# LSH attention and two expert layers on one core: q and k transposed side by side, hashed by three products a half, and placed by copies inside SBUF

## The chip, the cores and the metric

The kernel runs on one core of a Trainium2 chip. The metric is the device time of one execution in microseconds (us), the median of several runs; lower is better. Beside the runs one execution was profiled.

## The reference

The kernel computes an attention with a hashing mask and two mixture-of-experts layers behind it. The attention is what matters here. It has 2 x 8 = 16 heads, 768 positions and a head width of 64, all in float32:

```python
B, H, S, D = q.shape                     # 2, 8, 768, 64
q_bits = (np.einsum('bhsd,dk->bhsk', q, proj) > 0)     # proj: 64 x 6
k_bits = (np.einsum('bhsd,dk->bhsk', k, proj) > 0)
mask = q_bucket[:, :, :, None] == k_bucket[:, :, None, :]   # all 6 bits equal
scores = scale * np.matmul(q, k.transpose(0, 1, 3, 2))
scores = np.where(mask, scores, -1000000000.0)
attn = softmax(scores)                   # over the keys
out = np.matmul(attn, v)
```

Its result, 1536 tokens of 512 values, goes through two expert layers (8 experts each, the first with the two best experts of a token, the second with the best one).

## The kernel before

**Split values.** TensorE multiplies here in a float32 form of reduced precision (F32R). Where float32 exactness is wanted, a value is split into a high part (its rounded copy) and a low part (what is left), and the products high x high, high x low and low x high are summed.

**Operands of the scores.** Scores need q and k with the head width on the partitions. A head has four operand tiles of 128 x 768, in two sets (parity of the head): `q_hl` (rows 0 to 63 high part of q, rows 64 to 127 low part), `k_hh` (high part of k twice), `q_hb` and `k_lb` (rows 0 to 63 high part of q and low part of k; rows 64 to 75 the hash bits as large or tiny numbers, so that positions of different buckets get a huge negative score). One half of a score tile is two products: `q_hl` x `k_hh`, and `q_hb` x `k_lb` over 76 rows.

**Preparing a head.** `load_qk` on the SP queue brings k and q in twice each (four DMAs in 256-byte pieces), so that each is side by side with itself. Six units, listed in `PREP`, turn them: ("k", 0), ("q", 0), ("k", 1), ("q", 1), then ("bits", 0), ("bits", 1); the number is the half of the 768 positions. A k or q unit is three transposes of 128 x 128 on TensorE into a PSUM bank (`prep_unit`, L1024), a copy of the high part by ACT (`copy_unit`, L548) and the subtraction that gives the low part on DVE (`prep_unit`, L696). As k or q stands there twice, the bank has it in rows 0 to 63 and again in rows 64 to 127, so each engine writes every piece straight to the rows where it belongs; only the high part of q in `q_hl` is a copy by GpSimd (`q_copy`, L448). A bits unit is four hashing products into the bank (108 rows: the bits of k in rows 64 to 75, those of q in 96 to 107) and two comparisons on DVE.

**The head's steps.** A head has 6 tiles of 128 queries, one for each step j. In step j TensorE issues (L1096): the scores of tile j, the unit j of the next head, the weighing (`weigh`, probabilities x v) of the tile two back, and the transposes of the probabilities (`turn`) of the tile before. DVE (L752) finds the tile's maximum and the two scalars of its exponential (L722 to L728), does its part of the unit and every second time half of an evacuation; ACT (L579) does its part of the unit, the exponential of tile j, then the evacuations of the turned probabilities. The scores' banks and the operand sets are double.

**The SP queue** issues in its own order (L362 to L370), for each head: wait for the four transpose units, load q and k of the head after next; wait for the last weighing of the head before, load v. After every second head come `clear` twice and `clear_y`: zeros to tables in HBM, 2.6 MB in three DMAs. Semaphores: `qk_ld` loads landed, `prep_mm` a unit on TensorE done, `prep_cp` a high part copied, `prep_ev` a unit on DVE done, `q_top` GpSimd's copy done.

Of the kernel before, what the change touches and what calls it, by code (L numbers as in the profile page):

```python
# [5 lines left out]
P = 128  # L6
# [14 lines left out]
def lsh_attention_two_moes(nc, q, k, v, proj, moe_w_gate, moe_w_noise, moe_noise, moe_w1, moe_w2,  # L21
# [31 lines left out]
    with ctx:  # L53
# [16 lines left out]
        qraw = raw[:, 0:2].rearrange("p a t d -> p (a t d)").rearrange("p (t r d) -> p t r d", t=QT, d=D)  # L70
        kraw = raw[:, 2:4].rearrange("p a t d -> p (a t d)").rearrange("p (t r d) -> p t r d", t=QT, d=D)
# [12 lines left out]
        k_lb = [ring_part(3), ring_part(7)]  # L84
        probs = [work[:, i * S:(i + 1) * S] for i in range(2)]
# [27 lines left out]
        p_f = work[:, 0:2 * PW].rearrange("p (a b) -> p a b", a=2)  # L113
        p_h, p_l = (ring_part(8 + i)[:, 0:2 * PW].rearrange("p (a b) -> p a b", a=2) for i in range(2))
        p_k1 = ring_part(10)[:, 0:PW]
# [92 lines left out]
        prep_cp = sem("prep_cp")  # L208
        prep_ev = sem("prep_ev")
        q_top = sem("q_top")  # L210
# [81 lines left out]
        PREP = [("k", 0), ("q", 0), ("k", 1), ("q", 1), ("bits", 0), ("bits", 1)]  # L292
        U = len(PREP)
        assert QT == U

# [28 lines left out]
        def _(sp):  # L324
            def load_qk(h):
                for raw_rows, t in ((kraw, k), (qraw, q)):
                    for r in range(2):
                        sp.dma_start(raw_rows[:, :, r], head_rows(t, h)).then_inc(qk_ld, 16)

            def load_v(h, par):  # L330
                sp.dma_start(vraw[:, par], head_rows(v, h)).then_inc(v_ld[par], 16)

# [22 lines left out]
            sp.wait_ge(prep_mm, 4)  # L355
            load_qk(1)
            sp.wait_ge(pool_c, 1)
# [75 lines left out]
        def _(pool):  # L433
# [13 lines left out]

            def q_copy(h, par):  # L448
                for half in range(2):

                    pool.wait_ge(prep_cp, h * 4 + (2 * half + 2))
                    high = q_hb[par][0:D, cols(half)].bitcast(F32)
                    nc.gpsimd.tensor_tensor(q_hl[par][0:D, cols(half)], high, ones[0:D, 0:1].broadcast_to([D, HALF]),  # L453
                                            ALU.mult).then_inc(q_top, 1)

            q_copy(0, 0)
            over_heads(pool, lambda h, par: None if last(h) else q_copy(h + 1, 1 - par))
# [78 lines left out]
        def _(act):  # L536
# [7 lines left out]
            act.wait_ge(qk_ld, 64)  # L544
# [3 lines left out]
            def copy_unit(h, par, u):  # L548

                what, half = PREP[u]  # L550
                if what in ("k", "q"):
                    act.wait_ge(prep_mm, h * U + (u + 1))
                    to = k_hh[par] if what == "k" else q_hb[par]
                    nc.scalar.activation(to[:, cols(half)], prep_bank(h, u)[:, 0:HALF],  # L554
                                         ACT.Copy).then_inc(prep_cp, 1)
# [19 lines left out]

            for u in range(U):
                copy_unit(0, 0, u)

            def head(h, hp):  # L579
                for j in range(QT):  # L580
                    n = h * QT + j
                    if not last(h):
                        copy_unit(h + 1, 1 - hp, j)
# [75 lines left out]
        def _(dve):  # L659
# [23 lines left out]
            link(vec.tensor_scalar(bit_rule[:, 3:4], second[:], -2.0, 1.0, ALU.mult, ALU.add))  # L683
            link(vec.memset(p_f, 0.0))
            dve.wait_ge(proj_ld, 32)

            for side in range(2):
                neg, plus = (QB, QB + BITS) if side == 0 else (D + BITS, D)
                link(vec.tensor_scalar(p_f[:, side, neg:neg + BITS], praw[:], -1.0, None, ALU.mult))
                link(vec.tensor_copy(p_f[:, side, plus:plus + BITS], praw[:]))  # L690
            link(vec.tensor_copy(p_h, p_f))
            link(vec.tensor_tensor(p_l, p_f, p_h.bitcast(F32), ALU.subtract))
            link(vec.tensor_copy(p_k1[0:D, :], p_h[0:D, 1, :]))
            link(vec.tensor_copy(p_k1[D:P, :], p_l[D:P, 1, :]))

            def prep_unit(h, par, u):  # L696
                what, half = PREP[u]
                c = cols(half)
                bank = prep_bank(h, u)
                if what == "k":  # L700
                    dve.wait_ge(prep_cp, h * 4 + (u + 1))
                    ins = vec.tensor_tensor(k_lb[par][0:D, c], bank[0:D, 0:HALF],
                                            k_hh[par][0:D, c].bitcast(F32), ALU.subtract)
                elif what == "q":
                    dve.wait_ge(prep_cp, h * 4 + (u + 1))
                    ins = vec.tensor_tensor(q_hl[par][D:P, c], bank[D:P, 0:HALF],
# [603 lines left out]
```

## Time and profile before

| | |
|---|---|
| median of 3 runs | 1034.82 us (1034.65 to 1037.06) |
| profiled execution | 1035.75 us, its span 1033.9 us, mean granted clock 0.96 |
| TensorE matmuls busy | 936.5 us, 91% of the span |
| DVE, ACT, GpSimd busy | 587.9, 340.3, 410.1 us |
| attention | first scores at 16.95 us, last at 340.3 us |
| DMA | 158.3 MB, 153 GB/s over the span |

The profile is one execution. An instruction's row has its start from the span's start, its duration, engine, line and operands; PE is TensorE's matmul, PEld its weight load, DVE VectorE, ACT ScalarE, POOL GpSimd, SPq the queue of SyncE that issues DMAs. Brackets tell how long an engine sat idle before and what ended that. Matmul durations overlap, so starts are what to compare. The granted clock is TensorE's, 1.00 being 2.4 GHz and 0.50 being 1.2 GHz.

### The profile page before, as it was taken

What the parts mean: (1) busy time and instruction counts of PE and PEld (TensorE: products, weight loads), DVE (VectorE), ACT (ScalarE), POOL (GpSimd) and SP (SyncE); (2) the same over time, 40 slices, a digit from 0 to 9 for tenths busy, and PEclk for the clock granted to TensorE, in tenths of its full rate; (3) what the DMA queues carried; (4) which work ended last, traced back from release to release, by engine and by line L of the source; (5) the groups of instructions that cost most, each with busy time, mean ns of one, the idle gap of its engine ahead of it and who ended that gap; (6) DMA issues with size and microseconds to landing.
All of it is one profiled execution on the core that took longest, in us unless ns stands there. A gap on an engine that the chain in (4) does not pass through costs nothing. (4 is left out here: it accounts for less than half of the span.)

```text
span 1033.9 us, 19204 instructions
## 1 busy us (share of the span) xinstructions
PE 936.5 (91%) x5502; PEld 793.0 (77%) x5503; DVE 587.9 (57%) x1136; ACT 340.3 (33%) x548; POOL 410.1 (40%) x251
## 2 busy tenths in 40 slices
PE   6999999999999938999999999999854999999980
PEld 4889988988898726888888888888643788888860
DVE  5777777777777474544445544454367454444432
ACT  2655555565555410422121111120212134342000
POOL 1000000000000547966152433331955889896004
PEclk9999999999999967999999999999976999999995
DMA  8351543435514525655252534332765677774107
GB/s 264 95 156 38 147 138 70 139 89 124 142 38 171 203 98 207 238 191 189 75 181 84 170 102 141 122 131 87 231 210 189 216 239 254 234 252 147 47 31 243
DMA packets 116173, 158.31 MB, mean 153 GB/s; under 512 B 57904, under 2 KB 59952, under 8 KB 116144
## 3 DMA queue, kind: packets, MB, share of 16 engines
q1 hardware_dynamic: 83280, 70.37, 22.3%
q10 hardware_dynamic: 26624, 67.12, 19.9%
q0 software_dynamic: 6240, 20.45, 6.1%
q8 instruction: 16, 0.26, 0.1%
q14 instruction: 13, 0.11, 0.0%
HBM read 104.43 MB, written 53.48 MB: 153 GB/s over the span
## 5 line engine op out<-in xcount | busy, mean ns | idle before, releaser
L463 POOL TENSOR_TENSOR wring<-stage,wring 128x1024 f32 (+1 forms) x128 | 302.3, 2395 | 197.1 <-ACT wring L618 197.0
L618 ACT ACTIVATE wring<-stage 128x1024 f32 (+1 forms) x128 | 135.4, 1061 | 429.7 <-POOL wring L463 213.8
L1203 PE MATMUL bank<-wring,xT_hl 128*128 x352 | 142.7, 405 | 5.2 <-DVE xT_hl L936 5.2
L1083 PE MATMUL bank<-raw,work 128*128 128x64 f32 x1152 | 143.6, 275 | 3.2 <-ACT work L569 3.2
L1083 PEld LDWEIGHTS bank<-raw,work 128*128 128x128 f32 x1152 | 135.9, 191 | 12.9 <-issue 10.9
L1220 PE MATMUL bank<-wring,hT_hl 128*128 x352 | 141.6, 402 | 3.2 <-DVE hT_hl L955 3.2
L453 POOL TENSOR_TENSOR wring<-wring,ones 64x384 fp32r<-64x384 f32 x32 | 26.2, 819 | 287.3 <-ACT wring L554 287.3
L1205 PE MATMUL bank<-wring,xT_hl 128*128 x352 | 138.8, 394 | 0.0
L1204 PE MATMUL bank<-wring,xT_hl 128*128 x352 | 137.9, 392 | 0.0
L1222 PE MATMUL bank<-wring,hT_hl 128*128 x352 | 137.8, 391 | 0.0
L1221 PE MATMUL bank<-wring,hT_hl 128*128 x352 | 137.1, 390 | 0.0
L962 DVE COPY work<-bank 128x512 f32<-128x512 f32 x44 | 30.5, 694 | 178.2 <-PE bank L1222 168.5
L561 ACT ACTIVATE work<-bank,stat 128x768 f32<-128x768 f32 x96 | 95.2, 991 | 101.8 <-DVE stat L728 101.8
L722 DVE TENSOR_REDUCE stat<-bank 128x1 f32<-128x768 f32 x96 | 91.8, 956 | 59.7 <-PE bank L1060 58.5
L943 DVE TENSOR_SCALAR work<-bank 128x512 f32<-128x512 f32 x88 | 60.9, 692 | 108.2 <-PE bank L1205 108.2
L1203 PEld LDWEIGHTS bank<-wring,xT_hl 128*128 128x128 f32 x352 | 66.8, 190 | 18.6 <-issue 6.2
L1071 PE MATMUL bank<-ident,work 128*128 128x128 f32 x576 | 79.9, 275 | 0.6 <-ACT work L569 0.6
L1220 PEld LDWEIGHTS bank<-wring,hT_hl 128*128 128x128 f32 x352 | 66.1, 188 | 16.1 <-issue 3.7
L1205 PEld LDWEIGHTS bank<-wring,xT_hl 128*128 128x128 f32 x352 | 66.6, 189 | 14.8
L1222 PEld LDWEIGHTS bank<-wring,hT_hl 128*128 128x128 f32 x352 | 66.1, 188 | 14.7
L1204 PEld LDWEIGHTS bank<-wring,xT_hl 128*128 128x128 f32 x352 | 67.0, 190 | 13.0
L1221 PEld LDWEIGHTS bank<-wring,hT_hl 128*128 128x128 f32 x352 | 66.3, 188 | 12.7
(171 smaller groups left out, 1290.6 us busy)
## 6 DMA issues: line engine op xcount, KB each, us to landing
stage<-in_moe_w_dram ACTq DMA_DIRECT2D x128, 512.0 KB, 4.0
ys<-work SPq DMA_DIRECT2D x44, 256.0 KB, 3.4
work<-xs SPq DMA_DIRECT2D x40, 256.0 KB, 3.5
xs<-stage SPq DMA_DIRECT2D x7, 1024.0 KB, 4.5
ys<-stage SPq DMA_DIRECT2D x7, 1024.0 KB, 8.2
raw<-in_k_dram SPq DMA_DIRECT2D x32, 192.0 KB, 3.6
raw<-in_q_dram SPq DMA_DIRECT2D x32, 192.0 KB, 3.8
xs<-stage SPq DMA_DIRECT2D x7, 512.0 KB, 5.2
```

The lines of the kernel that those rows point to most:

```text
L463: nc.gpsimd.tensor_tensor(wring[:, bass.ds(at + DC * F, GW)], stage[:, j % STAGES, :], wring[:, bass.ds(at, GW)].bitcast(F32), ALU.subtrac ...
L561: nc.scalar.activation(probs[par].rearrange("p (b c) -> p b c", b=2), s_ps[par][:, :, 0:HALF], ACT.Exp, bias=stat[:, par, 2:3], scale=stat ...
L618: nc.scalar.activation(wring[:, bass.ds(parity * SLOT + high_at(j), GW)], stage[:, j % STAGES, :], ACT.Copy).then_inc(w_high, 1)
L722: vec.tensor_reduce(stat[:, par, 0:1], s_ps[par][:, :, 0:HALF], AX.XY, ALU.max).then_inc(s_max, 1)
L1071: ins = nc.tensor.transpose(pt_ps[:, half, i * P:(i + 1) * P], probs[par][:, c:c + P], ident[:])
L1083: ins = mm(o_ps[:, j * D:(j + 1) * D], probsT[j % 2][:, i * P:(i + 1) * P], vraw[:, hp, i], start=i == 0, stop=i == QT - 1)
L1203: mm(o, xT_hl[:, 0, c, :], wh, start=c == 0, stop=False)
L1204: mm(o, xT_hl[:, 0, c, :], wl, start=False, stop=False)
L1205: ins = mm(o, xT_hl[:, 1, c, :], wh, start=False, stop=c == DC - 1)
L1220: mm(y_ps[:], hT_hl[:, 0, c, :], wh, start=c == 0, stop=False)
L1221: mm(y_ps[:], hT_hl[:, 0, c, :], wl, start=False, stop=False)
L1222: ins = mm(y_ps[:], hT_hl[:, 1, c, :], wh, start=False, stop=c == FC - 1)
```

## The change

- q and k are loaded once each, side by side in `qk_raw` (q in columns 0 to 63, k in 64 to 127): two DMAs a head instead of four.
- One unit for each half transposes both: q comes to rows 0 to 63, k to rows 64 to 127. ACT copies the high parts to `qk_top`, DVE subtracts to `qk_rest`, each 128 x 768 and single, not double.
- A bits unit has three products of 128 rows, `p_h` x `qk_top`, `p_h` x `qk_rest`, `p_l` x `qk_top`, and one comparison of 44 rows into `k_lb`, which carries the bits of q along in rows 96 to 107.
- A head has four units (`U = 4`), in steps 0 to 3; steps 4 and 5 have none.
- Seven DMAs inside SBUF (`put`) on the SP queue place the pieces: six of 64 rows x 768 when both subtractions are done, one of 12 rows (the bits of q) when both comparisons are. `qk_put` counts them; the first scores of a head wait for all seven and for the head's four units.
- The SP queue's order for a head is: wait, six copies, q and k of the head after next, wait, seventh copy, wait, v. The clears stay behind every second head.
- GpSimd's `q_copy` is gone. The bits rule and the projections are laid out for the new rows (DVE, at the start).

```diff
-        qraw = raw[:, 0:2]...
-        kraw = raw[:, 2:4]...
+        qk_raw = raw[:, 0:2].rearrange("p a t d -> p (a t d)").rearrange("p (t x) -> p t x", x=2 * D)
+        qk_top = ring_part(11)
+        qk_rest = ring_part(12)
...
-        PREP = [("k", 0), ("q", 0), ("k", 1), ("q", 1), ("bits", 0), ("bits", 1)]
-        U = len(PREP)
+        U = 4
+        PUTS = 7
...
             def load_qk(h):
-                for raw_rows, t in ((kraw, k), (qraw, q)):
-                    for r in range(2):
-                        sp.dma_start(raw_rows[:, :, r], head_rows(t, h)).then_inc(qk_ld, 16)
+                for at, t in ((0, q), (D, k)):
+                    sp.dma_start(qk_raw[:, :, at:at + D], head_rows(t, h)).then_inc(qk_ld, 16)
...
+            def put(to, at, n, t, row):
+                sp.dma_start(to[at:at + n, :].bitcast(F32), t[row:row + n, :].bitcast(F32)).then_inc(qk_put, 16)
+
+            def put_split(h, par):
+                sp.wait_ge(prep_ev, h * U + 2)
+                put(q_hl[par], 0, D, qk_top, 0)
+                put(k_hh[par], 0, D, qk_top, D)
+                put(q_hl[par], D, D, qk_rest, 0)
+                put(k_hh[par], D, D, qk_top, D)
+                put(q_hb[par], 0, D, qk_top, 0)
+                put(k_lb[par], 0, D, qk_rest, D)
+
+            def put_bits(h, par):
+                sp.wait_ge(prep_ev, h * U + 4)
+                put(q_hb[par], D, 2 * BITS, k_lb[par], QB)
...
-            sp.wait_ge(prep_mm, 4)
+            put_split(0, 0)
             load_qk(1)
+            put_bits(0, 0)
...
+            def next_head(h, par):
+                put_split(h + 1, 1 - par)
+                load_qk(h + 2)
+                put_bits(h + 1, 1 - par)
+                sp.wait_ge(s_pv, h * QT + QT)
+                load_v(h + 2, par)
+
             with sp.Fori(0, (H - 2) // 2) as i:
                 for par in range(2):
-                    sp.wait_ge(prep_mm, i * (2 * U) + (U * par + U + 4))
-                    load_qk(i * 2 + (2 + par))
-                    sp.wait_ge(s_pv, i * (2 * QT) + QT * (par + 1))
-                    load_v(i * 2 + (2 + par), par)
+                    next_head(i * 2 + par, par)
                 for m in range(2):
                     clear(m, i * share[m], share[m])
                 clear_y(0, i * share[0], share[0])
+            put_split(H - 1, 1)
+            put_bits(H - 1, 1)
...
-            def copy_unit(h, par, u):
...
+            def top_part(h, u):
+
+                act.wait_ge(prep_mm, h * U + (u + 1))
+                nc.scalar.activation(qk_top[:, cols(u)], prep_bank(h, u)[:, 0:HALF], ACT.Copy).then_inc(prep_top, 1)
...
+                if u < 2:
+                    dve.wait_ge(prep_top, h * 2 + (u + 1))
+                    ins = vec.tensor_tensor(qk_rest[:, c], bank[:, 0:HALF], qk_top[:, c].bitcast(F32), ALU.subtract)
                 else:
                     dve.wait_ge(prep_mm, h * U + (u + 1))
+                    b = slice(D, PW)
+                    ins = vec.tensor_scalar(k_lb[par][b, c], bank[b, 0:HALF], bit_rule[b, 2:3], bit_rule[b, 3:4],
+                                            ALU.is_gt, ALU.mult)
...
                     for i in range(KH):
+                        ins = nc.tensor.transpose(bank[:, i * P:(i + 1) * P], qk_raw[:, half * KH + i], ident[:])
                 else:
-                    mm(to, p_k1, k_hh[par][:, c], start=True, stop=False)
-                    mm(to, p_h[0:D, 1, :], k_lb[par][0:D, c], start=False, stop=False)
-                    pe.wait_ge(q_top, h * 2 + 2)
-                    mm(to, p_h[:, 0, :], q_hl[par][:, c], start=False, stop=False)
-                    ins = mm(to, p_l[0:D, 0, :], q_hb[par][0:D, c], start=False, stop=True)
+                    to = bank[0:PW, 0:HALF]
+                    mm(to, p_h, qk_top[:, c], start=True, stop=False)
+                    mm(to, p_h, qk_rest[:, c], start=False, stop=False)
+                    ins = mm(to, p_l, qk_top[:, c], start=False, stop=True)
...
             def scores(n, j, h, hp):
+                if j == 0:
+                    pe.wait_ge(qk_put, h * (16 * PUTS) + 16 * PUTS)
+                    pe.wait_ge(prep_ev, h * U + U)
...
-                    if not last(h):
+                    if not last(h) and j < U:
                         prep_unit(h + 1, 1 - hp, j)
```

## Rows read from the trace of the kernel before

**Rows 1.** Busy us by stage: engine (instructions), granted clock, DMA share, GB/s; attention.
```profile
200.00:250.00 50.00, 49.66 (x379) 45.56 (x379) 38.15 (x80) 29.80 (x62) 4.10 (x5) 1.00 0.34 93
```

**Rows 2.** Groups of instructions, 20 to 420 us: busy us, mean ns, idle before.
```profile
L453 POOL TENSOR_TENSOR wring<-wring,ones 64x384 fp32r<-64x384 f32 x30 | 24.6, 819 | 278.9 <-ACT wring L554 278.9
...
L710 DVE TENSOR_SCALAR wring<-bank,bit_rule 12x384 fp32r<-12x384 f32 x30 | 20.2, 674 | 1.0
```

**Rows 3.** One line's instructions: duration ns, least, median, most.
```profile
L728 DVE SCALAR_TENSOR_TENSOR stat<-stat x96: 159/160/556, 20.7 to 341.7; 128x1 f32<-128x1 f32 x96
```

**Rows 4.** Timeline, one head: start, us, engine, line; each step's first score weights.
```profile
61.04 0.19 PEld L1059 LDWEIGHTS bank<-wring 128*128 128x128 f32 x1
...
64.03 0.19 PEld L1059 LDWEIGHTS bank<-wring 128*128 128x128 f32 x1
...
70.43 0.19 PEld L1059 LDWEIGHTS bank<-wring 128*128 128x128 f32 x1
...
74.50 0.19 PEld L1059 LDWEIGHTS bank<-wring 128*128 128x128 f32 x1
...
78.58 0.19 PEld L1059 LDWEIGHTS bank<-wring 128*128 128x128 f32 x1
...
81.59 0.19 PEld L1059 LDWEIGHTS bank<-wring 128*128 128x128 f32 x1
```

**Rows 5.** Timeline: the last hashing product's weight load, and the weighing behind it.
```profile
72.20 0.17 PEld L1048 LDWEIGHTS bank<-wring 64*108 64x108 f32 x1 [0.18 <-issue]
...
72.56 1.41 PEld L1083 LDWEIGHTS bank<-raw,work 128*128 128x128 f32 x12 [0.19 <-issue]
```

**Rows 6.** Timeline: exponentials, and the weighings' weight loads.
```profile
63.91 0.99 ACT L561 ACTIVATE work<-bank,stat 128x768 f32<-128x768 f32 x1 [1.03 <-DVE stat L728]
...
65.49 1.42 PEld L1083 LDWEIGHTS bank<-raw,work 128*128 128x128 f32 x12 [0.38 <-issue]
...
79.64 1.42 PEld L1083 LDWEIGHTS bank<-raw,work 128*128 128x128 f32 x12
...
81.08 0.99 ACT L561 ACTIVATE work<-bank,stat 128x768 f32<-128x768 f32 x1 [0.64 <-DVE stat L728]
```

**Rows 7.** Timeline of the SP queue: start, us of issue, what is issued.
```profile
63.67 0.37 SPq L331 DMA_DIRECT2D raw<-in_v_dram  x1
...
64.25 1.00 SPq L352 DMA_DIRECT2D xs<-stage  x2
...
65.43 0.97 SPq L348 DMA_DIRECT2D ys<-stage  x1
...
89.48 1.25 SPq L328 DMA_DIRECT2D raw<-in_k_dram  x2
```

**Rows 8.** Single microseconds, columns as in rows 1: clears, then loads; loads alone.
```profile
66.00:67.00 1.00, 1.00 (x12) 1.00 (x11) 0.93 (x4) 0.19 (x1) 0.00 (x0) 1.00 1.03 397
...
72.00:73.00 1.00, 1.00 (x6) 0.63 (x7) 0.90 (x4) 0.11 (x1) 0.00 (x0) 1.00 0.99 221
...
76.00:77.00 1.00, 1.00 (x6) 0.63 (x6) 0.90 (x4) 0.03 (x1) 0.00 (x0) 1.00 0.39 62
...
93.00:94.00 1.00, 1.00 (x9) 0.89 (x8) 0.93 (x3) 0.55 (x1) 0.00 (x0) 1.00 1.14 257
```

**Rows 9.** DMA issues by kind: count, KB each, median us to landing.
```profile
raw<-in_v_dram SPq DMA_DIRECT2D x16, 192.0 KB, 2.4
```

**Rows 10.** Timeline: the first score product's weight load.
```profile
16.95 0.29 PEld L1059 LDWEIGHTS bank<-wring 128*128 128x128 f32 x1 [0.33 <-issue]
```

**Rows 11.** Two-microsecond slices ahead of the experts, columns as in rows 1.
```profile
368.00:370.00 2.00, 0.86 (x7) 0.44 (x4) 0.28 (x1) 0.88 (x2) 0.00 (x0) 1.00 0.00 0
...
370.00:372.00 2.00, 0.00 (x0) 0.00 (x0) 0.84 (x4) 1.99 (x4) 0.00 (x0) 0.88 0.72 260
...
396.00:398.00 2.00, 1.31 (x3) 1.12 (x4) 0.37 (x1) 0.00 (x0) 1.58 (x2) 0.50 0.51 156
...
402.00:404.00 2.00, 2.00 (x10) 1.68 (x9) 0.69 (x1) 0.00 (x0) 1.39 (x3) 0.94 0.43 164
```

More of the change, by code:

```diff
@@ L112, in lsh_attention_two_moes @@
         PW = QB + 2 * BITS
-        p_f = work[:, 0:2 * PW].rearrange("p (a b) -> p a b", a=2)
-        p_h, p_l = (ring_part(8 + i)[:, 0:2 * PW].rearrange("p (a b) -> p a b", a=2) for i in range(2))
-        p_k1 = ring_part(10)[:, 0:PW]
+        p_f = work[:, 0:PW]
+        p_h, p_l = (ring_part(8 + i)[:, 0:PW] for i in range(2))
         wg_sb = [sb("wg0", [P, DC, 2 * E]), sb("wg1", [P, DC, E])]
@@ L446, in _ @@
             nc.gpsimd.iota(tri_in[:], [[1, E], [-1, E]], base=0, channel_multiplier=0, **io).then_inc(pool_c, 1)
[L448 to L457, printed above, removed]
             def low_part(g, parity, pieces=range(GRAN)):
@@ L543, in _ @@
             AHEAD = STAGES - 2
-            act.wait_ge(qk_ld, 64)
+            act.wait_ge(qk_ld, 32)
             for j in range(AHEAD):
                 load_piece(0, 0, j)
-            def copy_unit(h, par, u):
[L550 to L555, printed above, removed]
+            def top_part(h, u):
+                act.wait_ge(prep_mm, h * U + (u + 1))
+                nc.scalar.activation(qk_top[:, cols(u)], prep_bank(h, u)[:, 0:HALF], ACT.Copy).then_inc(prep_top, 1)
             def expo(n, par, j, hp):
@@ L574, in evacs @@
                     evac(n, j % 2, 1, pt_b)
-            for u in range(U):
-                copy_unit(0, 0, u)
+            for u in range(2):
+                top_part(0, u)
             def head(h, hp):
@@ L581, in head @@
                     n = h * QT + j
-                    if not last(h):
-                        copy_unit(h + 1, 1 - hp, j)
+                    if not last(h) and j < 2:
+                        top_part(h + 1, j)
                     expo(n, j % 2, j, hp)
@@ L683, in _ @@
             link(vec.tensor_scalar(bit_rule[:, 3:4], second[:], -2.0, 1.0, ALU.mult, ALU.add))
+            link(vec.tensor_copy(bit_rule[QB:P, 2:4], bit_rule[QB:P, 0:2]))
             link(vec.memset(p_f, 0.0))
             dve.wait_ge(proj_ld, 32)
[L687 to L690, printed above, removed]
+            for rows, neg, plus in ((slice(0, D), QB, QB + BITS), (slice(D, P), D + BITS, D)):
+                link(vec.tensor_scalar(p_f[rows, neg:neg + BITS], praw[rows, :], -1.0, None, ALU.mult))
+                link(vec.tensor_copy(p_f[rows, plus:plus + BITS], praw[rows, :]))
@@ L1024, in prep_unit @@
             def prep_unit(h, par, u):
-                what, half = PREP[u]
+                half = u % 2
                 if not first(h):
@@ L1053, in scores @@
                     pe.wait_ge(s_exp, n - 1)
+                if j == 0:
+                    pe.wait_ge(qk_put, h * (16 * PUTS) + 16 * PUTS)
+                    pe.wait_ge(prep_ev, h * U + U)
                 t = slice(j * P, (j + 1) * P)
                 for half in range(2):
-                    if j == 0:
-                        pe.wait_ge(prep_ev, h * U + (U - 1 + half))
                     o, c = s_ps[j % 2][:, half, 0:HALF], cols(half)
@@ L1089, in _ @@
             pe.wait_ge(pool_c, 9)
-            for u in range(4):
+            for u in range(2):
                 prep_unit(0, 0, u)
-            pe.wait_ge(dve_c, 20)
-            for u in range(4, U):
+            for u in range(2, U):
+                if u == 2:
+                    pe.wait_ge(dve_c, 19)
                 prep_unit(0, 0, u)
@@ L1099, in head @@
                     scores(n, j, h, hp)
-                    if not last(h):
+                    if not last(h) and j < U:
                         prep_unit(h + 1, 1 - hp, j)
```

35 lines of the change are left out of this document (5 added, 30 removed).

## The prediction, made before the changed kernel was run

> **What bounds the kernel now.** I read the busy time by stages first. In the attention stretch TensorE is busy for 49.66 of 50 us at full clock, while DVE has 38.15 and ACT 29.80 [rows 1]. So time is won only where TensorE's stream gets shorter, and only down to the next limit. The change touches the attention part alone; the two expert parts keep their instructions and merely start earlier or later.
>
> Then I read the timeline of one head. The weight loads of the first score product give the starts of the steps [rows 4]: step 1 from 61.04 to 64.03 (2.99 us), steps 2 and 3 together 6.40, step 4 4.07, step 5 4.08, step 0 of the next head 3.01, in all 20.55 us for a head. A step holds scores, one unit of preparation, the weighing of the tile two back and the turning of the tile before. Weighing and turning take 81.59 - 79.64 = 1.95 [rows 4, 6], so scores and a unit of three transposes take 78.58 to 79.64 = 1.06. A transpose unit alone is about 0.40 (the step of 3.01 without it would be 2.61). In steps 4 and 5 the unit is four hashing products, and 1.06 + 0.40 taken away from 4.07 leaves about 1.47 for it.
>
> A second limit lies just under the first: the loop through DVE and ACT. From the scores' start to their exponential 2.50 us pass (78.58 to 81.08), from an exponential's start to the weighing in the next step, where that waits for it, 1.58 (63.91 to 65.49), then 1.95 to the scores after [rows 4, 6]. Two steps can't take less than 2.50 + 1.58 + 1.95 = 6.03 us, however little TensorE has to do. That is 3.01 a step: today's transpose steps sit on both limits.
>
> **The change part by part.**
> *Transposes.* Six per head go (12 become 6), two units of 0.40. *Hashing.* A product there costs 72.56 - 72.20 = 0.36 [rows 5]; four become three per half, so a unit is about 1.12. TensorE's stream shrinks by 0.80 + 0.72 = 1.52 us a head. But the units now stand in steps 0 to 3 (0.40, 0.40, 1.12, 1.12), and 4 and 5 have none. With 2.61 + unit and the loop of 6.03 for each pair, the steps are 3.01, 3.02, 3.73, 3.73, 2.61 and 6.03 - 2.61 = 3.42: 19.52 us, against 20.55. The gain is 1.03 a head (bounds: 0.72 if the empty steps give nothing, 1.52 if the loop doesn't hold). Fifteen heads prepare a next one: 15.5 us (10.8 to 22.8).
>
> *GpSimd's copy and DVE's stalls.* The 0.82 us copies of q go [rows 2]. The small DVE operation ahead of the exponential takes 0.16 us in the median and 0.556 at most [rows 3]: in steps 1 and 3 it pays 0.4 more while such a copy runs. That pause ended in steps 2 and 4, which now have or had products in its place, so I count it at nothing further. ACT makes two copies a head fewer; of DVE's four hash comparisons of 0.67 a head [rows 2] two are left, and of its four subtractions two: less load on engines that aren't full.
>
> *The small copies.* Six DMAs per head move 64 rows of 3 KB each (197 KB), 1.18 MB in all, and a seventh 12 rows. They are issued by SP, whose queue is a line. Behind the first wait stand the six copies, then the q and k loads of the head after next, the wait for the hashes, the seventh copy, the wait for the weighing and the v load. A v load, 0.37 us of issue and 2.4 us to land [rows 7, 9], is the nearest price of one. In a head without clears there is room: copies can go after the second subtraction, about 6.0 us into the head, are through by 12.5, the loads by 14.3, the seventh copy, issued at about 13, lands near 15.5, and the next head's scores come at 19.5.
>
> In every second head it is different. SP has just issued 2.6 MB of clears (64.25 to 66.4) [rows 7] when the copies come up, and they queue behind them. The DMA bytes of this stretch end at about 76.3 [rows 8]: that is 18.2 us after the head's start at 58.03 (61.04 - 3.01). Of those bytes the change takes half of the q and k loads, 0.39 MB, at the 221 GB/s of that stretch 1.8 us, and adds the copies, P. With 0.8 us from the last bytes to the semaphore (an estimate: of a v load's 2.4 us its bytes take 0.9 at 221 GB/s, and some 0.7 pass ahead of the first), the seventh copy lands 17.2 + P after the head's start, and scores want it at 19.5. The stall is P - 2.3.
>
> P has no row in the trace: no large DMA there has 64 partitions, or goes from SBUF to SBUF. The clears, in 2 KB pieces, ran at 397 GB/s [rows 8]: P = 3.0, a stall of 0.7. The q and k loads, in 256-byte pieces, ran at 221 GB/s: P = 5.3, a stall of 3.0. I take 5.3, because each copy uses half of the partitions at both ends and six small DMAs follow one another. Clears precede seven heads' copies: 7 x 3.0 = 21 us (5 to 21). What is queued behind the wait on TensorE is everything, and DVE and ACT run dry behind it.
>
> The Trainium skill has a rule against this change: SBUF — State Buffer, "Door 1: The DMA port swizzle", says that 64 partitions reach only half of SBUF's ports and were measured at 196 GB/s, and that two transfers on the two halves serialize. No row here shows it; by that figure P would be 6.0, the stall 3.7 and this term 26.
>
> *The clock.* Before the experts TensorE stopped at about 369 and the granted clock fell from 2.4 to 1.2 GHz within the slice 370 to 372 (0.88 of full over it), some 2.5 us after the stop; it was still at half at 396 to 398, when work had resumed, and came back early in 402 to 404 [rows 11]. So a fall costs about half of 5.4 us, 2.7. A stall of 3 us is at the edge of it; I count two falls in seven, 5.4 us (0 to 19).
>
> *The start.* First scores came at 16.95 [rows 10]. Two of four loads go from the front (two are issued in 1.25 us [rows 7]), and the hashing needs no placed pieces; but scores now wait for the seventh copy, behind six others, two loads and its own landing of 2.4 us. I take +1 us, bounds -1 and +4. *Constants* on DVE: one link more, two fewer; hidden under the loads at the start.
>
> **Sum.** The profiled execution has 1035.75 us (span 1033.9, and 1.85 around it), 0.93 above the median of 1034.82. 1035.75 - 15.5 + 21 + 5.4 + 1 = 1047.65; less the 0.93 it is 1046.7, say 1047.
>
> **The rivals.**
> *The copies are hidden* (faster). With P = 3.0 the stalls sum to 5, no clock falls: 1034.82 - 15.5 + 5 + 1 = 1025. With P under 2.3 it is 1020. For it: the rate of the clears. The case turns at P = 4.4, where seven stalls of 2.1 and the start give back all 15.5; a P near that is the next case.
> *Break-even.* P of 3.9 to 4.7 (250 to 300 GB/s): stalls of 1.6 to 2.4, 1031.5 to 1037. For it: the loads without clears reach 257 GB/s in one of their microseconds [rows 8].
> *Every stall costs the clock too* (slower still). A P of 5.5 or more, stalls from 3.2, and a fall each time: 1034.82 + 21 + 19 + 1 - 15.5 gives 1060 and more. For it: the fall 2.5 us after a stop [rows 11]; against it: a wait of 3 us ends just as the clock would fall.
> *The start goes wrong*: that the seventh copy of head 0 lands behind the constants' small pieces would add 3 us more, which lies inside the other cases.
>
> **How the numbers follow.** Forecast case, stalls of 2.4 to 3.6 us with few falls: 0.45, 1040 to 1054. Hidden: 0.26. Break-even: 0.11. Clock falls too: 0.18. A measurement of this kernel can tell some 0.3% (3 us) from no change. Faster by more: 0.27. Within: 0.12. Slower: 0.61. The range leaves out the wholly hidden end (under 1024) and the worst of the clock case (over 1062).
>
> **What would show it.** Score starts 19.5 us apart in heads without clears; a wait of TensorE for DMA ahead of the first score product in heads 3, 5, ... 15 and nowhere else, some 3 us long; steps 4 and 5 of about 2.6 and 3.4; the copies' bytes at some 220 GB/s; granted clock below 1.00 in a few slices of the attention part. If TensorE waits for DMA in every head, my estimate of the uncrowded heads (4 us of room) is wrong; if it waits in none, P is. If the heads shorten by 1.5 rather than 1.0, the loop isn't the limit I take it for.

## The result and the profile after

| | before | changed |
|---|---|---|
| median | 1034.74 us (1034.05 to 1037.06) | 1055.03 us (1054.8 to 1056.87) |
| ratio | | 1.0196 (95%: 1.0176 to 1.0216) |
| profiled span | 1033.9 us | 1053.4 us |
| first score products | 16.95 us | 20.27 us |
| last step's scores (head 15, step 5) | 339.49 us | 360.89 us |
| head without a stall | 20.55 us | 18.28 us |

The changed kernel is 2% slower, although a head that isn't disturbed is 2.3 us shorter. The page of the changed kernel (span; busy time, share and instructions; the 40 slices of TensorE and of its clock; the group of the first score product, with what ended the idle time ahead of it):

```profile
span 1053.4 us, 18828 instructions
...
PE 922.6 (88%) x5374; PEld 801.8 (76%) x5375; DVE 537.1 (51%) x1071; ACT 323.3 (31%) x516; POOL 383.7 (36%) x219
...
PE   3989898898989873999999999999954899999980
...
PEclk9998898988989895999999999999977999999995
...
L1050 PE MATMUL bank<-wring 128*128 128x384 f32 x192 | 80.2, 418 | 34.3 <-DMA wring<-wring 32.3
```

and its waits (line, what it waited for: us in total, times, longest):

```profile
PE bank L1050 <- DMA wring<-wring: 32.3, 8, 9.6
```

TensorE is 88% busy where it had 91% and its clock has 8s in the attention slices where it had 9s. The score products of L1050 have waited 32.3 us for the copies inside SBUF, in eight places: 9.6 us ahead of the very first scores, the others ahead of heads 3, 5, 7, 9, 11, 13 and 15 (this list counts from the modelled ends of the matmuls; by the lengths of the steps the seven cost 26.1 us).

The weight loads of TensorE in head 3 of the changed kernel, step starts and one hashing unit (start, us, engine, line), which answer to [rows 4, 5]:

```profile
79.34 0.29 PEld L1050 LDWEIGHTS bank<-wring 128*128 128x128 f32 x1 [4.04 <-issue]
...
84.95 0.34 PEld L1050 LDWEIGHTS bank<-wring 128*128 128x128 f32 x1
...
88.97 0.19 PEld L1050 LDWEIGHTS bank<-wring 128*128 128x128 f32 x1
...
89.61 0.17 PEld L1036 LDWEIGHTS bank<-wring 128*108 128x108 f32 x1
89.78 0.17 PEld L1037 LDWEIGHTS bank<-wring 128*108 128x108 f32 x1
89.96 0.17 PEld L1038 LDWEIGHTS bank<-wring 128*108 128x108 f32 x1
```

Head 3's scores begin at 79.34, after 4.04 us without a weight load. Its steps 0 and 1 take 5.61 and 4.02 us: the weight loads of 0.29 and 0.34 us there are those of the half clock, 0.19 of the full one. From 88.97 the steps are normal. The three hashing products start 0.17 to 0.18 us apart, where [rows 5] had 0.36.

What SP issued around it, against [rows 7], and the DMA engines by the microsecond, against [rows 8] (the columns as there; the clock is third from the end, the last is GB/s):

```profile
63.19 0.99 SPq L366 DMA_DIRECT2D xs<-stage  x2
...
65.66 7.89 SPq L332 DMA_DIRECT2D wring<-wring  x6
...
75.23 0.85 SPq L332 DMA_DIRECT2D wring<-wring  x1
```

```profile
65.00:66.00 1.00, 1.00 (x11) 1.00 (x11) 0.92 (x3) 0.52 (x1) 0.00 (x0) 1.00 1.04 399
...
70.00:71.00 1.00, 1.00 (x10) 0.87 (x9) 0.83 (x2) 0.10 (x1) 0.00 (x0) 1.00 1.04 383
...
73.00:74.00 1.00, 0.73 (x7) 0.67 (x7) 0.90 (x1) 0.66 (x2) 0.00 (x0) 1.00 0.98 243
...
75.00:76.00 1.00, 0.55 (x6) 0.31 (x3) 0.41 (x1) 1.00 (x3) 0.00 (x0) 1.00 1.03 219
76.00:77.00 1.00, 0.00 (x0) 0.00 (x0) 0.14 (x1) 0.03 (x1) 0.00 (x0) 0.96 1.26 185
77.00:78.00 1.00, 0.00 (x0) 0.00 (x0) 0.00 (x0) 0.00 (x0) 0.00 (x0) 0.50 1.28 213
...
87.00:88.00 1.00, 1.00 (x11) 1.00 (x9) 0.93 (x4) 0.49 (x1) 0.00 (x0) 0.92 0.00 0
...
91.00:92.00 1.00, 1.00 (x11) 1.00 (x11) 0.93 (x3) 0.45 (x1) 0.00 (x0) 1.00 0.89 277
...
93.00:94.00 1.00, 1.00 (x10) 1.00 (x8) 0.84 (x1) 0.40 (x2) 0.00 (x0) 1.00 0.94 243
```

The clears start at 63.19, the six copies are issued from 65.66 on, the seventh at 75.23, and it landed when the scores began, at 79.34. The clears' microseconds, 65 to 71, have 373 to 399 GB/s; behind them, until 78, the rate is 185 to 329, so here the copies' and loads' bytes come after the clears'. TensorE stopped at about 75.5, and the clock fell within slice 76 (0.96 on the mean of that slice) and stood at 0.50 from then on until slice 87. In the quiet head 3, microseconds 90 to 95, the copies ran at 243 to 277 GB/s, in the last two with the loads beside them. Six of the seven waits look alike: step 5 of heads 2, 4 ... 12 takes 7.00 to 7.25 us, where 3.17 is normal. In head 14 it takes 5.43.

**Where the time went**, added from the step starts of both traces: fifteen heads at 18.28 and not 20.54 give 33.9 us; the first scores come 3.3 later; the seven waits cost 26.1; the half clock behind them 26.0 (steps 0 and 1 of heads 3 to 13: 22.9; head 15: 3.1); the part behind the attention is 1.9 shorter. 3.3 - 33.9 + 26.1 + 26.0 - 1.9 = 19.6, and the spans differ by 19.5.

### The profile page after: what moved, and what is told of

The parts are those of the page before. It is cut to its first block and busy times, and to the rows that moved or that the text cites. A ratio compares the mean times of both kernels' runs of the same rounds, so it can differ in the third digit from the quotient of the medians.

```text
span 1053.4 us, 18828 instructions
## 1 busy us (share of the span) xinstructions
PE 922.6 (88%) x5374; PEld 801.8 (76%) x5375; DVE 537.1 (51%) x1071; ACT 323.3 (31%) x516; POOL 383.7 (36%) x219
## 5 line engine op out<-in xcount | busy, mean ns | idle before, releaser
L624 ACT ACTIVATE wring<-stage 128x1024 f32 (+1 forms) x128 | 135.3, 1060 | 429.6 <-POOL wring L473 218.0
L1074 PEld LDWEIGHTS bank<-raw,work 128*128 128x128 f32 x1152 | 149.0, 204 | 12.2 <-ACT work L575 10.4
L1074 PE MATMUL bank<-raw,work 128*128 128x64 f32 x1152 | 151.8, 285 | 4.5 <-ACT work L575 4.5
L1050 PE MATMUL bank<-wring 128*128 128x384 f32 x192 | 80.2, 418 | 34.3 <-DMA wring<-wring 32.3
L1062 PE MATMUL bank<-ident,work 128*128 128x128 f32 x576 | 84.5, 286 | 1.1 <-ACT work L575 1.1
L1195 PEld LDWEIGHTS bank<-wring,xT_hl 128*128 128x128 f32 x352 | 66.5, 189 | 18.6 <-issue 6.3
```

The source lines that it names most:

```text
L624: nc.scalar.activation(wring[:, bass.ds(parity * SLOT + high_at(j), GW)], stage[:, j % STAGES, :], ACT.Copy).then_inc(w_high, 1)
L1062: ins = nc.tensor.transpose(pt_ps[:, half, i * P:(i + 1) * P], probs[par][:, c:c + P], ident[:])
L1074: ins = mm(o_ps[:, j * D:(j + 1) * D], probsT[j % 2][:, i * P:(i + 1) * P], vraw[:, hp, i], start=i == 0, stop=i == QT - 1)
L1195: mm(o, xT_hl[:, 0, c, :], wh, start=c == 0, stop=False)
```

## The experiments

My theory after the result: the seventh copy comes late in every second head since the clears' bytes are moved ahead of the copies, and each such wait is paid a second time through the clock. The rivals are that the copies are slow by themselves, that only the line on SP's queue matters, and for the larger gain, that fewer products explain it all. Runs 5 and 6, the first of the wide copies and the start in order (8) ran on another chip, where the kernel before takes 1062 us; the steps that the edits leave alone last as long there (run 5: 3.00, 3.40 and 2.99 for steps 1 to 3), so for these I compare steps of the attention and ratios only. The kernels of 2 to 7 and 9 were executed once each, so I read them by their steps; the two in 8 and the one in 1 have four times.

**1. The clears elsewhere (clears_moved).**

```diff
                 load_qk(h + 2)
                 put_bits(h + 1, 1 - par)
+                if clears:            # every second head
+                    clears()
                 sp.wait_ge(s_pv, h * QT + QT)
                 load_v(h + 2, par)
...
-                for m in range(2):
-                    clear(m, i * share[m], share[m])
-                clear_y(0, i * share[0], share[0])
```

> The changed kernel with one edit: the 2.6 MB of clears of every second head are issued after that head's seventh copy and ahead of the wait for the weighing, not after the v load, so that they don't stand in front of the next head's copies. Theory (the copies are late because they queue behind the clears): the seven stalls of about 4.0 us at heads 3, 5 ... 15 go, and with them the seven stretches of half clock behind them (steps 0 and 1 of those heads 5.6 and 4.2 us, not 3.0 and 3.0, 3.8 us together). Heads are 18.3 us apart, span about 1053.4 - 7 x 7.8 = 999 us. Rival (the copies themselves, 64 partitions wide, are too slow, or the line of copies and loads is): heads with stalls stay as they are, about 1053. Second rival (clears and copies only change places: the clears now delay the loads of v and the copies of the odd head): stalls move to other heads, 1030 or more.

Median 1003.29 us (1000.88 to 1004.1), ratio to before 0.9693 (0.9677 to 0.9709), span 999.1. All heads from 2 on are 18.27 to 18.30 us apart, without a stall. SP's queue and the waits of TensorE for copies:

```profile
49.87 0.86 SPq L332 DMA_DIRECT2D wring<-wring  x1
50.95 1.07 SPq L366 DMA_DIRECT2D xs<-stage  x2
...
62.29 4.44 SPq L332 DMA_DIRECT2D wring<-wring  x6
```

```profile
PE bank L1054 <- DMA wring<-wring: 9.3, 2, 8.1
```

The seventh copy (49.87) is followed by the clears, whose last issue ends at about 53.3, and the next head's copies are issued from 62.29. The two waits left are the start and 1.2 us ahead of head 1. The theory holds to the microsecond (999 expected), and this version beats both kernels by 3 and 5%.

**2. The same clears at the same time from another queue (clears_by_gpsimd).**

```diff
-                for m in range(2):
-                    clear(m, i * share[m], share[m])
-                clear_y(0, i * share[0], share[0])
...
+            with pool.Fori(0, (H - 2) // 2) as i:
+                pool.wait_ge(s_pv, i * (2 * QT) + 2 * QT)
+                for m in range(2):
+                    nc.gpsimd.dma_start(xs_d[m]..., zeros...).then_inc(xs_zp, 16)
+                nc.gpsimd.dma_start(ys_d[0]..., zeros...).then_inc(ys_zp, 16)
```

> The changed kernel with the clears of the loop issued by GpSimd, on its own queue, at the same moment as before (after the last weighing of the head before). The bytes and the moment are the same, only the line in which they stand is another. Theory (a line on one queue): copies pass the clears; as both share the 16 DMA engines the copies take at most twice their 4.6 us and the stalls shrink from 4.0 to under 1, span 999 to 1010. Rival (what counts is the DMA engines' work in that stretch, 2.6 + 1.2 + 0.4 MB, whoever issues it): stalls stay near 4.0, span near 1053.

Here my theory fell and its rival won: one time of 1065.8 us, span 1064.2. Step 5 of heads 2 to 12 takes 7.3 to 8.4 us (head 14: 6.0). DMA queues from 50 to 100 us (packets, MB, share of the engines; then KB each and us to landing), and TensorE by 5 us behind head 2:

```profile
q1 hardware_dynamic: 6100, 4.21, 37.6%
q0 software_dynamic: 688, 2.62, 14.2%
...
ys<-stage POOLq DMA_DIRECT2D x1, 1024.0 KB, 13.9
```

```profile
75.00:80.00 5.00, 0.72 (x5) 0.49 (x3) 0.56 (x1) 0.70 (x3) 0.00 (x0) 0.90 0.68 161
80.00:85.00 5.00, 5.00 (x24) 4.90 (x24) 2.08 (x6) 1.57 (x3) 0.00 (x0) 0.50 0.00 0
```

The clears stand on their own queue (q0), yet they need 13.9 us to land and the copies beside them are no sooner through. So the delay doesn't need the line on SP's queue: with the clears out of it, the DMA engines have the same bytes to move in this stretch (their share is 0.9 to 1.06 from 65 to 78), and the seventh copy comes no sooner, even somewhat later, as the clears start more slowly on GpSimd's queue (146 to 256 GB/s in microseconds 63 to 66); no other queue was tried. That doesn't make the prediction's "they queue behind them" wrong for the changed kernel, whose rates show the clears' bytes first; and the order within the line can count, as run 4 will show. Moving the bytes in time helped, moving them to another queue didn't.

**3. TensorE kept at work through the stall (warm_in_stall).**

```diff
                 if j == 0:
+                    if hp == 1:
+                        for i in range(22):
+                            mm(s_ps[0][:, 0, 0:HALF], q_hl[0][:, 0:P], k_hh[0][:, 0:HALF], start=True, stop=True)
                     pe.wait_ge(qk_put, h * (16 * PUTS) + 16 * PUTS)
```

> The changed kernel with 22 products of 384 columns put on TensorE ahead of the wait for the copies in odd heads (into the score bank that is free then, results overwritten), so that TensorE works through the stall. Theory (half of the price of a stall is the clock): the stalls' ends stay where they are, the granted clock stays 1.00, steps 0 and 1 of heads 3, 5 ... 15 take 3.0 and 3.0, not 5.6 and 4.2: 7 x 3.8 = 27 us less, head 1 pays up to 3.1 us more for products without a stall, span about 1030. Rival (those steps are long because DVE and ACT have run dry or the DMA is behind): they stay at 5.6 and 4.2 and the span grows to about 1056.

1034.55 us, span 1032.8. TensorE from 78.8 us (start, us, line):

```profile
78.81 4.09 PE L1047 MATMUL bank<-wring 128*128 128x384 f32 x22
82.73 0.39 PE L1053 MATMUL bank<-wring 128*128 128x384 f32 x1
...
85.69 0.42 PE L1053 MATMUL bank<-wring 128*128 128x384 f32 x1
```

The 22 products without use fill the 3.9 us of the wait, head 3 begins with steps of 2.99 and 2.99, and so do the other odd heads, within 0.03. Step 5 of the even heads remains at 6.95 to 7.31, in head 0 too, where no wait was to be filled. The 22 products alone take 3.85 us, so they lengthen heads 0 and 14, whose waits were shorter, by 2.9 and 1.5 us; the clock's 26.0 less these and 0.6 for a later start give 21.0, and the span is 20.6 us shorter. This brings the changed kernel to the time of the kernel before: the clock was half of what the waits cost.

**4. The seventh copy ahead of the loads (bits_before_loads).**

```diff
                 put_split(h + 1, 1 - par)
-                load_qk(h + 2)
                 put_bits(h + 1, 1 - par)
+                load_qk(h + 2)
```

> The changed kernel with the seventh copy issued ahead of the loads of q and k of the head after next. Theory: in the crowded heads the seventh copy no longer waits for 0.39 MB of 256-byte pieces, 1.7 us; the stalls shrink from 4.0 to 2.3 us and some of the clock falls behind them go with that, span 1053.4 - 12 = 1041 if every fall stays, 1015 if every one goes. Rival (the loads don't delay the copy, the clears and the six copies alone do): no change, 1053.

1045.76 us, span 1044.0. Step 5 of heads 2 to 12 takes 5.34 to 6.60 us, 5.67 on the mean, and 7.13 in the changed kernel: 1.5 us less, near the 1.7 that I gave it. Head 14, which has no loads behind its copies, is as it was (5.46 against 5.43), which is what the theory wants. The clock still fell in heads 3 to 13 (step 0 at 4.6 to 5.6), in four of the six behind a wait of 2.2 us, and in heads 3, 5 and 11 it stayed low for longer, as q and k now came late for step 0. TensorE's weight loads around head 5's start and the clock by the microsecond (third from the end):

```profile
123.15 0.19 PEld L1050 LDWEIGHTS bank<-wring 128*128 128x128 f32 x1 [2.22 <-issue]
```

```profile
124.00:125.00 1.00, 0.65 (x6) 0.53 (x6) 0.84 (x1) 0.00 (x0) 0.00 (x0) 1.00 0.00 0
125.00:126.00 1.00, 1.00 (x9) 1.00 (x7) 0.86 (x6) 0.87 (x2) 0.00 (x0) 0.57 0.00 0
```

The clock was still full when work resumed at 123.15 and fell at about 125.1, some 4 us after the stop. It was so behind all the waits of 2.2 us here, head 15's too. In the changed kernel it had fallen 1.4 to 1.8 us after the stop, also in head 14's wait of 2.3 us. So a wait of 2.2 us was long enough, though the fall could come when it was over.

**5. The kernel before with full rows (before_full_rows).**

```diff
                     mm(to, p_k1, k_hh[par][:, c], start=True, stop=False)
-                    mm(to, p_h[0:D, 1, :], k_lb[par][0:D, c], start=False, stop=False)
+                    mm(to, p_k1, k_hh[par][:, c], start=False, stop=False)
                     pe.wait_ge(q_top, h * 2 + 2)
                     mm(to, p_h[:, 0, :], q_hl[par][:, c], start=False, stop=False)
-                    ins = mm(to, p_l[0:D, 0, :], q_hb[par][0:D, c], start=False, stop=True)
+                    ins = mm(to, p_h[:, 0, :], q_hl[par][:, c], start=False, stop=True)
```

> The kernel before, its loads, transposes, GpSimd copies and waits as they are, with the two hashing products of 64 rows in each half (low part of k, and low part of the projection) replaced by repeats of the two 128-row products beside them. What it leaves out are those two small terms of the hash, so that a bit near zero can come out wrong; four products remain. Theory (the 64-row products keep the next weight load from running beside a product, and that is why four took 1.47 us): a unit takes 4 x 0.175 = 0.70, steps 4 and 5 take 3.3 and not 4.08, a head 19.0 and not 20.54, span 1033.9 - 15 x 1.55 = 1011. Rival (108 columns of weights, or four products in a row, make them slow, 0.36 each whatever the rows): no change, 1034. By this run the changed kernel's gain is split into its parts: what the rows gave and what fewer products and transposes gave.

Weight loads of one unit of step 4, and the weighing behind it:

```profile
66.19 0.17 PEld L1044 LDWEIGHTS bank<-wring 128*108 128x108 f32 x1
66.37 0.17 PEld L1045 LDWEIGHTS bank<-wring 128*108 128x108 f32 x1
66.54 0.17 PEld L1047 LDWEIGHTS bank<-wring 128*108 128x108 f32 x1
66.71 0.17 PEld L1048 LDWEIGHTS bank<-wring 128*108 128x108 f32 x1
66.94 1.42 PEld L1083 LDWEIGHTS bank<-raw,work 128*128 128x128 f32 x12
```

The loads start 0.17 us apart and the weighing's comes 0.75 us after the first, where the prediction had 1.47 for the unit from the steps of [rows 4]; steps 4 and 5 take 3.35, a head 19.19. Loads, transposes and copies are as before, so, taken in this order, 1.36 of the 2.27 us a head come from the products' rows and only 0.91 from all else that was removed.

**6. One product of 64 rows in the version with the clears moved (one_product_of_64_rows).**

```diff
-                    ins = mm(to, p_l, qk_top[:, c], start=False, stop=True)
+                    ins = mm(to, p_l[0:D], qk_top[0:D, c], start=False, stop=True)
```

> The version with the clears moved, with the third hashing product (low part of the projection) cut from 128 to 64 rows; it leaves out that term for k. Theory (a change between 64 and 128 rows makes the weight load wait): the unit goes from 0.52 to about 0.96 us, because both its own load and the weighing's behind it wait, steps 2 and 3 go from 3.18 to 3.6, a head from 18.28 to 19.15, span 999 + 13 = 1012. Rival (half the rows cost no more): 999.

```profile
67.57 0.17 PEld L1040 LDWEIGHTS bank<-wring 128*108 128x108 f32 x1
67.74 0.17 PEld L1041 LDWEIGHTS bank<-wring 128*108 128x108 f32 x1
68.18 0.17 PEld L1042 LDWEIGHTS bank<-wring 64*108 64x108 f32 x1 [0.26 <-issue]
68.53 1.42 PEld L1078 LDWEIGHTS bank<-raw,work 128*128 128x128 f32 x12 [0.19 <-issue]
```

The 64-row load waits 0.26 us and the 128-row one behind it 0.19 (in brackets): 0.96 us for the unit, as expected. The head takes 19.06 us and not 18.28. The rival is out from both sides. What is shown is the cost of a 64-row product between 128-row ones; no run has several 64-row products in a row, so whether the rows or the change of rows costs stays open. The same trace shows what doesn't cost: the score products alternate 128 and 76 rows 0.18 us apart.

**7. The copies' width (copies_of_128_rows, wide_copies_in_the_crowd).** The same edit in the version with the clears moved and in the changed kernel:

```diff
-                put(q_hl[par], 0, D, qk_top, 0)
-                put(k_hh[par], 0, D, qk_top, D)
-                put(q_hl[par], D, D, qk_rest, 0)
-                put(k_hh[par], D, D, qk_top, D)
+                put(q_hl[par], 0, P, qk_top, 0)
+                put(k_hh[par], 0, P, qk_rest, 0)
```

> The version with the clears moved, with four of the six copies of 64 rows replaced by two of 128 rows that move the same bytes (high parts to one operand tile, low parts to the other; it leaves out the right placing, so the scores are wrong). The six copies ran at 243 to 277 GB/s in a quiet head of the changed kernel. Theory (64 rows reach half of the ways into SBUF): the microseconds of the 128-row copies show 350 to 400 GB/s. Rival (copies inside SBUF run at some 260 GB/s whatever their rows): 240 to 280 throughout. The span doesn't tell: the copies are hidden in this version, only the first scores may come 1 us sooner; 997 to 1000.

> The changed kernel, clears where it has them, with four of the six copies of 64 rows replaced by two of 128 rows over the same bytes (it leaves out the right placing, so the scores are wrong). In the quiet version such copies ran at 356 to 402 GB/s where the 64-row ones had 214 to 292. Theory (stall = time of the clears + time of the copies + loads - what the head has room for): 0.79 MB at 380 and not 250 GB/s is 1.1 us less, the stalls of 4.0 us shrink to 2.9, and some clock falls go: step 5 of heads 2, 4 ... 14 takes 6.1 and not 7.1 us. Rival (copies behind the clears run at the clears' rate anyway, whatever their rows): step 5 stays at 7.1.

Microseconds with copies, last column GB/s, first of 128 rows, then of 64 rows in the version with the clears moved:

```profile
44.00:45.00 1.00, 1.00 (x11) 1.00 (x11) 0.90 (x4) 0.00 (x0) 0.00 (x0) 1.00 1.01 402
...
63.00:64.00 1.00, 1.00 (x11) 1.00 (x11) 0.57 (x1) 1.00 (x3) 0.00 (x0) 1.00 0.99 381
```

```profile
64.00:65.00 1.00, 1.00 (x11) 1.00 (x11) 0.89 (x3) 0.65 (x1) 0.00 (x0) 1.00 1.00 267
...
66.00:67.00 1.00, 1.00 (x10) 1.00 (x9) 0.94 (x1) 0.19 (x1) 0.00 (x0) 1.00 0.96 246
```

402 and 381 against 267 and 246, with the DMA engines' share near 1.00 in both (second from the end), so SP's issues aren't what holds the 64-row ones back. The wide copies also carry twice the bytes each and stay on their own rows, so rows, size and the way from one half of the rows to the other changed together. The Trainium skill, in SBUF — State Buffer, "Door 1: The DMA port swizzle", says that 64 partitions reach only half of SBUF's ports; this case agrees that they are slower, but 64-row copies in a row, with their ends partly in different halves, moved some 250 GB/s here, not the 196 that the Trainium skill gives. In the crowd the wide copies cut step 5 of heads 2 to 12 to 5.75 to 6.23 us, 5.97 on the mean against 7.13: 1.2 us shorter, where 1.1 was expected. Head 15's wait is down to 0.5, and the span is 1031.0. The clock didn't fall in heads 11 and 15, was low for less long in 5 and 9 and for longer in 7. Head 11's wait was 2.6 us, longer than those of run 4 that brought a fall, so the length of a wait alone doesn't tell. In this one step the stalls shrank by as much as P.

**8. The start (start_in_order) and the first clears (clears_at_ends).** In the version with the clears moved, the loads of v, the gates and the noise go behind head 0's seventh copy; in a second step the first 4.6 MB of clears go behind the last head's copies:

```diff
             put_split(0, 0)
             load_qk(1)
             put_bits(0, 0)
+            load_v(0, 0) ... noise          # 6 DMAs, from the front
             sp.wait_ge(pool_c, 1)
-            clear(...), clear_y(...)        # 4 DMAs
...
             put_bits(H - 1, 1)
+            clear(...), clear_y(...)
```

> The version with the clears moved, and at the start the loads of v, of the gates and of the noise issued behind head 0's seventh copy and not ahead of its six copies. First scores came at 16.95 us before, 20.27 in the changed kernel, 18.64 in the version with the clears moved. Theory (these small pieces stand in the copies' way on the DMA engines at the start): first scores at 16 to 17, 2 us less, about 1001 at the median. Rival (the weights' first two pieces and the copies' own chain set it): no change within 0.5 us, 1003.

> The version with the clears moved and the start in order, and the first 4.6 MB of clears, which stood in the queue between head 0's seventh copy and head 1's copies, issued behind the copies of the last head. In the start-in-order version TensorE waited 4.8 us ahead of head 1 and ran steps 0 and 1 of it at half clock (5.6 and 4.2 us). Theory (that wait is the same mechanism as the seven of the changed kernel: clears' bytes ahead of a head's copies): it goes, head 1 has steps of 3.0 and 3.0, and the seven microseconds come back: attention's last score step starts at about 17.9 + 15 x 18.3 + 14.5 = 307, against 308.1 in the version with the clears moved. Rival (head 1 waits for the loads of v and of the gates that were put ahead of it): the wait of 4 to 5 us stays. Against the version with the clears moved the median is 0 to 3 us less, ratio to before 0.966 to 0.970.

The first step brought the first scores to 17.90, not to 16 or 17, and as profiles of kernels with one and the same start have them anywhere from 18.6 (run 1) to 21.0 (run 4), nothing can be read from that. At head 1 it lost: 4.8 us of wait and 5.61 and 4.23 us for its steps 0 and 1. Its ratio to before on its chip is 0.975 (0.9733 to 0.9766). With the first clears at the end that wait is gone, head 1 has 3.00 and 2.99, and the last step's scores come at 306.33, against 308.08. The median is 1001.89 us, ratio 0.9685 (0.9662 to 0.9708); against 0.9693 that is no difference that can be told. The start stays open: TensorE still waits 7.4 us for the seventh copy of head 0, and I didn't take its chain apart.

**9. GpSimd's copy twice, in the kernel before (gpsimd_copy_twice).**

```diff
                                             ALU.mult).then_inc(q_top, 1)
+                    nc.gpsimd.tensor_tensor(ring_part(11)[0:D, cols(half)], high, ...).then_inc(q_twice, 1)
+                    pool.wait_ge(q_twice, h * 2 + half + 1)
```

> The kernel before with GpSimd's copy of the high part of q made twice, the second time to unused memory. Theory (GpSimd's copy holds up DVE's small operation ahead of the exponential and so step 2, 3.40 us where 2.99 would do): the second copy meets other DVE operations of the same steps, the subtraction and the output scaling; step 2 grows by up to 0.8 us, a head from 20.54 to 20.6 to 21.4, span 1034 to 1046. Rival (step 2 is long because of the scaling of the output on DVE, not because of GpSimd): steps stay at 2.99, 3.40, 2.99.

```profile
63.63 0.82 POOL L454 TENSOR_TENSOR wring<-wring,ones 64x384 fp32r<-64x384 f32 x1 [12.55 <-ACT wring L558]
...
63.92 0.55 DVE L732 SCALAR_TENSOR_TENSOR stat<-stat 128x1 f32<-128x1 f32 x1
...
64.42 0.82 POOL L456 TENSOR_TENSOR wring<-wring,ones 64x384 fp32r<-64x384 f32 x1
64.50 0.56 DVE L710 TENSOR_TENSOR wring<-bank,wring 64x384 fp32r<-64x384 f32 x1
...
65.09 0.56 DVE L753 TENSOR_TENSOR x_sb<-bank,rinv 128x384 f32 x1
```

Steps stayed at 2.99, 3.40, 2.99, which was the rival's number, but the rows show that the doubling didn't test the theory. DVE's small operation, begun at 63.92 while the first copy ran, ends at 64.47, just behind it, and not after 0.16 us; the second copy meets only the subtraction (64.50) and the scaling (65.09), both with one input from PSUM, and they take the same 0.56 as without a copy. The doubling couldn't tell the two apart. The changed kernel, which has no GpSimd copy, can:

```profile
L724 DVE SCALAR_TENSOR_TENSOR stat<-stat x96: 159/159/163, 23.1 to 363.1; 128x1 f32<-128x1 f32 x96
```

At most 163 ns, where [rows 3] had 556. The scaling is still there and step 2 has lost its pause, so it was GpSimd's: step 2 takes 3.17 us, near the 2.61 of a step without a unit and 0.52 of the hashing unit together.

## Why the prediction was right, and where it wasn't

The forecast was 1047, measured are 1055; the direction and the mechanism came out, from terms that were wrong in size on both sides. That the number came so near is luck: the gain was 18.4 us larger than forecast, and the stalls (5.1), the clock (20.6) and the start (2.3) cost 28 more, less 1.9 behind the attention, for which there was no term.

- *What bounds the kernel.* Right: TensorE's stream and, close under it, the loop. With units gone from steps 4 and 5 these took 2.76 + 3.19 = 5.95 us in head 3; the loop's floor was put at 6.03, 0.1 too high. The loop holds, since step 5's weighing waits for ACT:

```profile
99.32 1.42 PEld L1074 LDWEIGHTS bank<-raw,work 128*128 128x128 f32 x12 [0.59 <-ACT work L575]
```

- *Transposes and hashing: 15.5 us, measured 33.9.* The step that failed is "four become three per half, so a unit is about 1.12". A unit takes 0.52. I took 0.36 for a product from [rows 5] without asking why it was twice a score product of the same 384 columns; the row showed it, 64x108 in the shape and a load that began only 0.18 us late. Runs 5 and 6 show that 64-row products between 128-row ones are the cause. The change ends it and I counted only the products it drops. With 0.52 for 1.12 in steps 2 and 3 the prediction's own sum of a head gives 18.32, and 18.28 was measured: the rest of that sum came out.
- *Where the stalls are.* Right: ahead of heads 3, 5 ... 15 and in no quiet head. The release at 22.4 us after the start of head 2 (79.34 - 56.99) is the 17.2 + 5.3 = 22.5 of the sum.
- *P.* 5.3 was taken; at the quiet head's 243 to 277 GB/s it is about 4.6. The range of 3.0 to 5.3 held it. With 4.6 the sum would give a release at 21.8; where the other 0.5 us lies in the crowded stretch was not taken apart, so part of the agreement is luck. (That two transfers on the two halves serialize is stated by the Trainium skill in SBUF — State Buffer, "Can I just issue two DMAs to hit both halves?", not in the section that the prediction names; no run here tests it.)
- *Size of a stall: 3.0, measured 3.9* (26.1 in all, not 21). The copies were no later than I said; the heads are 1.2 us shorter than my 19.5, so scores ask for them sooner. A gain I missed came back as a stall.
- *The clock: two falls of 2.7, measured six of 3.8 and one of 3.1.* This term, 5.4 against 26.0, is the largest miss on the slow side. The clock fell 1.4 to 1.8 us after TensorE stopped, not 2.5 as in [rows 11], and behind waits of 2.2 us too (run 4). A fall also lasted longer than the 5.4 us read there: the clock was at half for 10.2 us in heads 3 to 13 and for 6.8 in head 15. The rival "every stall costs the clock too" is what happened; its 1060 comes out 5 us over the measured time, as the missed gain of hashing is larger than what it still lacked in stalls, clock and start.
- *The start: +1, measured +3.3*, inside its bounds of -1 and +4; other profiles of the same start have 1.7 to 4.0 (runs 1 and 4).
- *That copies wait in SP's line* is what the changed kernel's rates show, but run 2 shows that they are as late without that line. What counts is the bytes that the DMA engines have to move by then.

## What to carry to other kernels

A step that leaves the critical engine and lands on the DMA engines must be counted in the stretch where these are fullest, with all bytes that are due there, whichever queue issues them; here 2.6 MB of clears, issued some 11 us earlier in the head's time or not, decided between 2% slower and 3% faster. A wait on TensorE of 2 us or more is to be priced with the half clock behind it, which doubled it here; in these traces it came behind every wait of 2.2 us or more between the attention's heads but one (run 7). And where a product takes twice its neighbour's time for the same columns, ask for the cause before costing by that row.

## What the runs showed of the hardware

- TensorE: products of 384 columns start 0.175 us apart when all have 128 rows, 0.36 when 128 and 64 alternate; the next weight load starts 0.18 to 0.26 us late then. 128 and 76 rows alternate at 0.18.
- The granted clock fell 1.4 to 1.8 us after TensorE stopped in the changed kernel, and behind waits of 2.2 us some 4 us after the stop, with work resumed (run 4). In head 3 it came back 7.8 us after work had resumed (79.34 to slice 87). 3.8 us were lost in each of heads 3 to 13. Products without use in the wait avoided it (run 3).
- DMA inside SBUF: in microseconds with copies alone, 64-row copies of 197 KB moved 244 to 292 GB/s, 128-row ones of 393 KB 356 to 402. SP needs 0.65 us to issue one of 64 rows in a quiet head, 1.3 behind the clears (six in 7.89); a v load 0.37.
- DVE's small operation with its inputs in SBUF lasted until GpSimd's copy was over (0.55 us, where it takes 0.16); two operations with one input from PSUM took 0.56 us beside a copy as without one.
